# The first product of a channel MLP by Strassen's algorithm in Winograd's form, its weights streamed pair by pair

## The reference

```python
# 1 attention over 2 x 8 heads with a hash mask  -> x [2, 768, 512]
# 2 _moe_ref
mixed = np.real(fft(fft(x, axis=1), axis=2));  u = x + mixed
un = (u - mean(u)) / sqrt(var(u) + 1e-6)
x  = u + np.maximum(un @ w_ch1, 0) @ w_ch2          # w_ch1 [512, 2048], w_ch2 [2048, 512]
# 3 _moe2_ref
h = gelu(x @ w_in);  a, v = h[..., :512], h[..., 512:]
v_n = layernorm(v) * g_ln
v_s = einsum('ts,bsd->btd', w_sg, v_n) + b_sg[None, :, None]
out = x + (a * v_s) @ w_out
```

## Time and profile before

| | |
|---|---|
| median of 3 runs | 742.23 us (742.17 to 742.39) |
| the profiled execution | 741.96 us, of which the span in the profile is 739.9 |
| TensorE busy | 729.6 us, 99% |
| VectorE, ScalarE, GpSimd busy | 395.2, 308.5, 284.8 us |

### The profile page before, as it was taken

One profiled execution on the slowest core, in us unless ns is written; L12 is line 12 of the kernel. 1 busy time (PEld: TensorE's weight loads), 2 busy tenths in 40 slices (PEclk: granted clock), 3 DMA queues, 4 the chain that ended last, 5 costly groups with the idle time before them and its releaser, 6 DMA issues.

```text
span 739.9 us, 11871 instructions
## 1 busy us (share of the span) xinstructions
PE 729.6 (99%) x3993; PEld 604.4 (82%) x3993; DVE 395.2 (53%) x629; ACT 308.5 (42%) x593; POOL 284.8 (38%) x292
## 2 busy tenths in 40 slices
PE   8999999999999999999999999999999999999998
PEld 8866666666766899999999999999899887888886
DVE  6977787777876798412221241213113696248633
ACT  4878887888884544111111111112124452025301
POOL 4188888888897500960000000000032254004400
PEclk9999999999999999999999999999999999999999
DMA  4433433433332302700000000000031000010001
GB/s 97 99 84 90 95 90 73 101 76 89 84 77 80 123 2 69 273 1 1 0 0 0 0 0 0 0 0 1 1 129 58 14 1 1 28 58 0 0 14 71
DMA packets 60118, 36.63 MB, mean 50 GB/s; under 512 B 44292, under 2 KB 52664, under 8 KB 59576
## 3 DMA queue, kind: packets, MB, share of 16 engines
q1 hardware_dynamic: 59512, 32.79, 16.4%
q0 software_dynamic: 576, 3.43, 1.3%
HBM read 27.03 MB, written 3.15 MB: 41 GB/s over the span
## 4 chain that ended last, share of the span: by engine, by line
PE 91%; DVE 4%; ACT 1%; issue 1%; POOL 1%; DMA 1%; SPq 0%; DVEq 0%; POOLq 0%; ACTq 0%
PE PS L692 87%; DVE mneg L1495 1%; PE PS L716 1%; PE PS L1085 1%; PE PS L1125 1%; PE PS L985 1%; PE PS L831 1%; PE PS L1053 1%; DMA ops<-mrow 0%; DVE ops L1466 0%; DVE ops L1487 0%; DVE ops L1460 0%; ACT ops L1169 0%; DMA pj<-in_proj_dram 0%; ACT E L1185 0%
## 5 line engine op out<-in xcount | busy, mean ns | idle before, releaser
L1757 DVE SCALAR_TENSOR_TENSOR hL<-PS,hH 128x384 fp32r<-128x384 f32 x64 | 35.7, 558 | 201.5 <-ACT hH L1387 201.5
L692 PE MATMUL PS<-ops 98*128 98x384 f32 (+1 forms) x576 | 134.7, 359 | 2.3 <-DVE mneg L1495 1.0
L692 PEld LDWEIGHTS PS<-ops 98*128 98x128 f32 (+1 forms) x576 | 95.1, 189 | 43.2 <-ACT E L1185 19.8
L1387 ACT ACTIVATE hH<-PS 128x384 fp32r<-128x384 f32 x64 | 31.4, 491 | 224.8 <-PE PS L692 224.8
L1495 DVE TENSOR_REDUCE mneg<-PS 128x1 f32<-128x768 f32 x96 | 91.5, 956 | 30.4 <-PE PS L692 29.8
L551 POOL TENSOR_TENSOR esum<-esum,E 128x768 f32<-128x768 f32 x56 | 102.4, 1829 | 2.8 <-ACT E L1185 0.3
L1185 ACT ACTIVATE E<-PS 128x384 f32<-128x384 f32 x192 | 83.5, 487 | 37.2 <-PE PS L692 35.0
L692 PE MATMUL PS<-unTH,W1L 128*128 128x384 f32 x256 | 86.4, 337 | 0.0
L692 PE MATMUL PS<-unTH,W1H 128*128 128x384 f32 x256 | 86.2, 337 | 0.0
L692 PE MATMUL PS<-unTL,W1H 128*128 128x384 f32 x256 | 86.0, 336 | 0.0
L692 PE MATMUL PS<-W2H,hL 128*128 128x512 f32 x192 | 75.9, 395 | 0.0
(11 more groups left out here) (193 smaller groups left out, 1412.7 us busy)
## 6 DMA issues: line engine op xcount, KB each, us to landing
ops<-ops SPq DMA_DIRECT2D x30, 192.0 KB, 3.0
W1R<-in_moe_w_ch_dram SPq DMA_DIRECT2D x16, 256.0 KB, 2.9
W2R<-in_moe_w_ch_dram SPq DMA_DIRECT2D x4, 1024.0 KB, 6.9
qk<-in_k_dram SPq DMA_DIRECT2D x32, 96.0 KB, 2.5
qk<-in_q_dram SPq DMA_DIRECT2D x32, 96.0 KB, 2.6
vn<-in_v_dram SPq DMA_DIRECT2D x32, 96.0 KB, 2.5
out_dram<-X SPq DMA_DIRECT2D x12, 256.0 KB, 2.0
WsgR<-in_moe_w_sg_dram SPq DMA_DIRECT2D x1, 2304.0 KB, 8.2
```

What stands on the lines that cost most here:

```text
L692: return pe.matmul(dst, lhs, rhs, start=start, stop=stop, **kw)
L1387: act.activation(M1["hH"][:, f % 2, :], PS[:, f % 2, 0:HALF], ACT.Relu).then_inc(hhi_done, 1)
L1757: dve.scalar_tensor_tensor(M1["hL"][:, f % 2, :], PS[:, f % 2, 0:HALF], 0.0, rd(M1["hH"][:, f % 2, :]), ALU.max, ALU.subtract).then_inc(hl ...
```

## The change

The first product of the MLP, `un @ w_ch1`, is taken with quarters: the 512 input features in two halves, the 2048 hidden features in two halves (block i and block i + 8 make pair i), and the 768 tokens of a batch in two halves. A pair of blocks and a batch make a 2 x 2 by 2 x 2 product of quarters, which takes 7 products (P1 to P7) instead of 8, each 2 steps of `mm3`, 6 matmuls of 384 columns. There are 16 pairs (8 for each batch, `NP`). Four signed sums of weight quarters (`weight_sums`, GpSimd) and four of token quarters (T1, T2 on VectorE, `token_differences`; T3, T4 on GpSimd, `token_sums`) are formed ahead of the products and split like all operands. Four results C11, C21, C12, C22 come out of products that are accumulated in two PSUM banks, with copies of partial sums by ScalarE (`keep_part`), two additions by VectorE (`side_quarter`) and one by GpSimd (`last_quarter`). The second product is as before, 4 x 9 matmuls for a pair, done one pair later, between the products of the next.

```diff
+            def pair(n):
+                later = [lambda quarter=quarter: second(n - 1, quarter) for quarter in LATER] if n else [lambda: None] * 4
+                product(n, P1)
+                product(n, P2)
+                later[0]()
+                product(n, P6)
+                product(n, P7)
+                later[1]()
+                product(n, P5)
+                product(n, P4)
+                later[2]()
+                product(n, P3)
+                if 1 <= n <= T:
+                    pe.wait_ge(pre_done, 2 * n + 2)
+                    un_transposes(T + n - 1, SIDE_BANK)
+                later[3]()
```

ScalarE's order in a pair; `next_un` rounds a token quarter of batch 1 in pair 7 alone:

```diff
+            for n in range(NP):
+                keep_part(n, P1, 0)
+                next_un(n, 0, P1)
+                next_un(n, 1, P2)
+                keep_part(n, P6, 1)
+                next_un(n, 2, P6)
+                keep_part(n, P7, 2)
+                if n + 1 < NP:
+                    weights_hi(n + 1)
+                next_un(n, 3, P7)
+                hidden_hi(n, C11)
+                keep_part(n, P5, 3)
+                w2_upper(n)
+                next_un(n, 4, P5)
+                hidden_hi(n, C21)
+                next_un(n, 5, P4)
+                hidden_hi(n, C12)
...
+                next_un(n, 6, P3)
+                hidden_hi(n, C22)
```

VectorE's and GpSimd's:

```diff
+            for n in range(NP):
+                if n == PAIRS - 1:
+                    token_differences(1)
+                side_quarter(n, C11)
+                next_un(n, 0)
+                next_un(n, 1)
+                next_un(n, 2)
+                if n + 1 < NP:
+                    weights_lo(n + 1)
...
+                next_un(n, 3)
+                hidden_lo(n, C11)
+                side_quarter(n, C21)
+                next_un(n, 4)
+                hidden_lo(n, C21)
+                next_un(n, 5)
+                hidden_lo(n, C12)
+                if n == PAIRS:
+                    channel_residual(0, 0, 4 * (PAIRS - 1) + 3)
+                next_un(n, 6)
+                hidden_lo(n, C22)
+                if n == PAIRS:
+                    channel_residual(0, 1, 4 * (PAIRS - 1) + 4)
...
+            for n in range(NP):
+                if n == PAIRS - 1:
+                    token_sums(1)
+                if n + 1 < NP:
+                    weight_sums(n + 1)
+                w2_lower(n)
+                last_quarter(n)
```

A product waits for the one whose bank it continues, and in the first pair of a batch for its token quarter:

```diff
+                if step == P1:
+                    pe.wait_ge(w1_lo, 3 * n + 3)
+                    if n:
+                        pe.wait_ge(hlo_done, 4 * (n - 1) + 3)
...
+                elif step == P7:
+                    pe.wait_ge(pre_done, 2 * n + 1)
+                else:
+                    pe.wait_ge(part_done, 4 * n + {P6: 1, P5: 2, P4: 3, P3: 4}[step])
+                if n % PAIRS == 0:
+                    pe.wait_ge(utl_done, 7 * b + UN_ORDER[b].index(k) + 1)
```

The weights are no longer prepared during attention. W1 and W2 blocks of a pair are loaded two pairs ahead, once for each batch. Those of pair 0 are summed and split during the Fourier mix of batch 0: `weight_sums(0)` and `first_weights_lower` on GpSimd, and on ScalarE:

```diff
                 if b + 1 < B:
+                    weights_hi(0)
                     fold_hi(2 * b + 2)
                     fold_hi(2 * b + 3)
```

More of the change, by code:

```diff
@@ L678, in _ @@
                                        ALU.pow).then_inc(rs2_done, 1)
[L679 to L681 removed]
+                scale_gate(b * T + T - 1, T - 1)
+                if b == 0:
+                    for t in range(KT):
                         pool.wait_ge(wout_hi, t + 1)
@@ new lines, in second @@
+            def second(n, quarter):
+                b, i, s = n // PAIRS, n % PAIRS, n % 2
+                f, block = int(quarter in (C21, C22)), int(quarter in (C12, C22))
+                pe.wait_ge(hlo_done, 4 * n + quarter + 1)
+                pe.wait_ge(w2_lo, n + 1)
+                if i == 0 and f == 0:
+                    if b:
+                        pe.wait_ge(x_upd, NT + T)
+                    else:
+                        pe.wait_ge(x_upd, NT)
+                        pe.wait_ge(ut_done, T)
@@ new lines, in keep_part, with hidden_hi @@
+            def keep_part(n, step, i):
+                bank = SIDE_BANK if step == P7 else CHAIN_BANK
+                act.wait_ge(p_rdy, 7 * n + step)
+                if i >= 2 and n:
+                    act.wait_ge(pre22_done, n)
+                copy(M1["part"][:, i, :], PS[:, bank, 0:HALF]).then_inc(part_done, 1)
+            def hidden_hi(n, quarter):
+                if quarter == C12:
+                    act.wait_ge(p_rdy, 7 * n + P3)
+                    src = PS[:, CHAIN_BANK, 0:HALF]
+                else:
+                    if quarter == C22:
+                        act.wait_ge(pre22_done, n + 1)
+                    else:
+                        act.wait_ge(pre_done, 2 * n + quarter + 1)
+                    src = M1["pre"][:, min(quarter, 2), :]
+                if n:
+                    act.wait_ge(y_rdy, 4 * (n - 1) + LATER.index(quarter) + 1)
+                act.activation(M1["hH"][:, quarter, :], src, ACT.Relu).then_inc(hhi_done, 1)
@@ L1394, in mlp_block @@
                         cols = slice((c % 2) * DM, (c % 2 + 1) * DM)
                         act.wait_ge(win_in, 16)
-                        copy(M2["WinH"][:, c // 2, cols], R1["WinR"][:, c // 2, cols]).then_inc(win_hi, 1)
-                    if not more and f >= FT - 2:
-                        act.wait_ge(wout_in, 16)
-                        for t in range((f - FT + 2) * KT // 2, (f - FT + 3) * KT // 2):
-                            copy(M2["WoutH"][:, t, :], R2["WoutR"][:, t, :]).then_inc(wout_hi, 1)
@@ L1413, in gate_hi @@
                 copy(M2["VH"][:, j, :], M2["vr"][:, j % 3, :]).then_inc(vh_done, 1)
-            with act.Fori(0, B) as b:
+            for b in range(B):
                 for j in range(T):
@@ new lines, in weights_lo, with side_quarter @@
+            def weights_lo(n):
+                s = n % 2
+                for i in range(3):
+                    rows = W1_PARTS[i][0]
+                    dve.wait_ge(w1_hi, 3 * n + i + 1)
+                    dve.tensor_tensor(M1["W1L"][:, s, rows, :, :], w1_source(s, i), rd(M1["W1H"][:, s, rows, :, :]),
+                                      ALU.subtract).then_inc(w1_lo, 1)
+            def side_quarter(n, quarter):
+                dve.wait_ge(p_rdy, 7 * n + (P2 if quarter == C11 else P4))
+                dve.wait_ge(part_done, 4 * n + quarter + 1)
+                dve.tensor_tensor(M1["pre"][:, quarter, :], PS[:, SIDE_BANK, 0:HALF], M1["part"][:, quarter, :],
+                                  ALU.add).then_inc(pre_done, 1)
@@ new lines, in hidden_lo, with channel_residual @@
+            def hidden_lo(n, quarter):
+                dve.wait_ge(hhi_done, 4 * n + (C11, C21, C12, C22).index(quarter) + 1)
+                src = PS[:, CHAIN_BANK, 0:HALF] if quarter == C12 else M1["pre"][:, min(quarter, 2), :]
+                dve.scalar_tensor_tensor(M1["hL"][:, quarter, :], src, 0.0, rd(M1["hH"][:, quarter, :]),
+                                         ALU.max, ALU.subtract).then_inc(hlo_done, 1)
+            def channel_residual(b, block, after):
+                dve.wait_ge(y_rdy, after)
+                for c in range(TH):
+                    N = b * T + block * TH + c
+                    dve.tensor_tensor(X[:, N, :], PS[:, y_bank(block, c), :], X[:, N, :], ALU.add).then_inc(x_upd, 1)
@@ L1785, in _ @@
             transformed_lo(1, 1, 1)
+            for n in range(TH, T):
+                normalise(n)
             flipped(1)
```

536 lines of the change are left out of this document (310 added, 226 removed).

## The result

The changed kernel takes 761.8 us (median; 758.0 to 762.7), the kernel before 742.3 on the same chip: 1.0252 times as long, 95% interval 1.0216 to 1.0288. It is 2.5% slower. The profiled execution took 761.2 us, 759.1 of them the span, 19.2 us more than that of before.

A forecast was written before the change was run, and what follows sets the result against it. TensorE, busy 99% of the span, was taken to bound the kernel. Waits of 29.1 us less 17.3 saved made it 11.8 slower: 741.96 to 753.8 profiled, so 754.0 median, range 741 to 763.

The forecast's parts named there:

- The likeliest case: The whole kernel: the forecast itself, waits as priced, 746 to 759 us; chance 0.52.
- the second rival: TensorE's clock falls in the gaps, pair 0's products running at 1.2 GHz: up to 5 us more, 759; chance 0.18.
- (a): Mix of batch 0: GpSimd's weight sums and split take turns with VectorE; 4.3 us lost, bounds 0 and 7.4.
- (b): Mix of batch 1: more statistics and normalisations on VectorE before the last GL and flips; 1.2 us, bounds 0 and 3.6.
- (c): Entry to the pairs: P1 waits for T1, T2, T3 and the first lower half; 2.3 us, bounds 0.5 and 4.6.
- (d): Pair 0: products wait behind seven lower halves and turns with GpSimd, lasting 18.0 us; 10.5 lost, bounds 7.5 and 12.
- (e): Pair 1: statistics and aggregations on VectorE stand ahead of the `side_quarter` P7 wants; 2.0 us, bounds 0 and 4.3.
- (f): Pair 7: batch 1's token operands, with turns, delay ScalarE and P1 of pair 8; 4.0 us, between 1.0 and 6.7.
- (g): Pair 9: batch 0's last three residuals end after `second` wants their banks; 1.4 us, bounds 0 and 2.
- (h): Gated MLP: VL and two w_sg splits make a stand of 4.3, replacing 0.9; 3.4 us lost, bounds 1 and 5.
- The first rival: VectorE and GpSimd turns do not happen or fall in slack: waits of 16.2 us, 741.1; chance 0.20.
- The third: Rival that every pair waits, C12's hL coming later than its cover: 7.5 us more over 15 pairs, 761; chance 0.07.

The follow-up runs named there:

- x_fill2: Changed kernel with idle matmuls, each no longer than its wait, in TensorE's waits of pair 0, pair 1 and ahead of the gated MLP's mixing: 756.2 us, 1.0177.
- x_early_b: Changed kernel with pair 0's weights loaded and summed in the attention, their GpSimd split delayed until VectorE has folded batch 1: 754.5 us, 1.0165.
- x_early: Changed kernel with pair 0's weights loaded, summed and split during the attention instead of in the mix of batch 0: 759.4 us, 1.0232.
- x_order: Changed kernel with pair 0's token halves made in the order the products use them, VectorE's first quarter and ScalarE's first copy between: 757.0 us, 1.0187.
- x_sums1: Changed kernel with GpSimd's sums of pair 1's weights right behind batch 0's reciprocal deviation instead of in pair 0: 760.7 us, 1.0236.
- x_swap: Changed kernel with GpSimd's sums of pair 8's weights ahead of batch 1's token sums in pair 7: 759.5 us, 1.023.
- x_pair7: x_swap with VectorE's lower halves 2 and 3 of batch 1's tokens behind pair 7's third lower quarter, 4 to 6 behind the fourth: 754.3 us, 1.0168.
- x_best: Changed kernel with edits of x_early_b, x_order, x_swap, x_pair7, a later mixing wait, earlier pair 1 sums, and idle matmuls in pairs 0 and 1: 736.51 us, 0.9921.

## Why the prediction came out as it did

It named 754.0 us, with 741 to 763 as range and slower at 0.77; 761.8 lies in the range, 7.8 above the number. The likeliest case (746 to 759) was not enough by itself: the second rival, the clock, happened on top of it. That the range held is in part luck: without the 3.5 us more that the change saved (below) the time would have been 765.3. Term by term, each measured from starts in the changed kernel's trace; "clock" is the part that was matmuls at the lower level:

| term | forecast | measured | of it clock |
|---|---|---|---|
| attention | 0 | 1.2 | |
| (a) mix of batch 0 | 4.3 | 4.2 | |
| (b) mix of batch 1 | 1.2 | 1.0 | 0.9 |
| (c) entry | 2.3 | 1.9 | |
| (d) pair 0 | 10.5 | 11.9 | 1.0 |
| (e) pair 1 | 2.0 | 3.0 | 1.3 |
| (f) pairs 7 and 8 | 4.0 | 8.9 | 3.6 |
| (g) pair 9 | 1.4 | 1.7 | |
| (h) gated MLP | 3.4 | 6.0 | 2.5 |
| lost | 29.1 | 39.8 | 9.3 |
| saved | 17.3 | 20.8 | |
| net | 11.8 | 19.0 (the profiled executions: 19.2) | |

How the middle column comes about: the first group of the mix starts at 262.77 in place of 261.56 (attention). z0L ended 5.4 us later, less 1.2 (a). The second transform of batch 1 ends at 307.7 in place of 300.0, less 1.2, 4.2 and 1.4 for twelve transposes that moved there (b). P1 of pair 0 at 309.59, less 307.7 (c). The pairs, from the starts above: 328.88 - 309.59 less 7.4 (d), 347.79 - 328.88 less 15.92 (e), 467.34 - 427.43 less 2 x 15.49 (f), 484.54 - 467.34 less 15.49 (g). The stand of 4.4 less 0.9, and 2.5 behind it (h). The clock part, in (d), (e) and (h), is what x_fill2 took away; in (f) it is what remains beside the waits. In (b) it is the time from z0L's end (285.88) to the group that it releases (286.90), less the 0.1 us that this takes in x_early_b.

- **(a) and (c): right in mechanism and size.** z0L ended 5.4 us later than in the earlier trace rows, 1.2 of them from the attention; x_early_b brought z0L 4.6 us forward, and x_early showed that it is the meeting that costs, wherever it takes place. In (c) P1 starts 4.6 us after the sixth tile's copy (309.59, with T1 at 304.99), as forecast; no experiment tried it.
- **(b): the right number by luck.** TensorE has no wait in the mix of batch 1. From its first group to its end it takes 20.8 us (286.90 to 307.7) in place of 19.4 (280.59 to 300.0), and 1.4 of that are the twelve transposes. The later GL and flips cost nothing; the 1.0 us is almost all slow matmuls behind the stand of (a), at the 0.50 of 284 to 287 us.
- **(d): right, with a wrong share.** Pair 0 was to last 18.0 us and lasted 19.3, 18.3 with the clock held up (x_fill2). Of what is beyond its matmuls, x_order took 4.1 us away by order (up to 1.0 of it clock), and x_sums1 showed 1.2 us for the sums' turns; the forecast had put some 5 us on turns with GpSimd. Those with T3 and T4 were not tried by themselves. Two sizes in the sum missed in opposite directions: P7 starts 9.5 us after P1 (319.11) where 10.7 was forecast, and from P7 to P1 of pair 1 it takes 9.8 us (8.8 with the clock held up) where 7.3 was.
- **(e): right in size, wrong in cover.** In the changed kernel no wait for the statistics shows in pair 1; its 3.0 us are slow matmuls. With the clock held up (x_fill2) the pair is 1.7 us too long and waits of 0.56 and 0.28 us for pre appear. The slow matmuls had hidden the late VectorE.
- **(f): too small.** The waits were 2.76 + 2.59 = 5.35 us against 4.0, inside the bounds. ScalarE was the late one, as forecast, but VectorE's row was as late right behind it (x_swap), and its halves ahead of its quarters were the cause (x_pair7).
- **(h): the stand was forecast at 4.3 and measured 4.37 us;** what was missing is the 2.5 us behind it.
- **The clock: the step that failed is that it stood as a rival to the forecast, with at most 5 us and in pair 0 alone.** It came with the forecast's own stands, at four places, and much of it lies not between them but in the full stretches behind them: 9.3 us, most of the 10.7 by which the loss exceeds the 29.1 of the forecast. The Trainium skill, "TensorE: Matmul & The Clock Gate", section "HAM oscillation — how this bites in real kernels", tells that the work after a gap starts at the lower clock; the windows above agree (0.50 from 329 to 335 us, TensorE busy throughout).
- **Saved: too small by 3.5 us.** 64 blocks of before took 4.19 us each, 268.2; the 16 pairs take 15.49 each without transposes, 247.8, and not 16 times 15.7. The matmuls start 1% closer together: a product group and a `second` group take 2.09 and 2.04 us in place of 2.11 and 2.08. Why was not tried; it hid part of the miss.
- **The attention's 1.2 us** were not forecast. A wait for the DMA of mrow at 42.75 us is 1.09 in place of 0.21, and it is in x_best too (1.1). The change only removed transfers there. Its cause stays open.
- The first rival (no turns) fell: Y took 3.15 us beside GpSimd. The third fell: pairs 2 to 6 have no wait. That the queues can be put in an order in which, with idle matmuls in what waits are left, the saving outweighs the rest is what x_best shows.

## What to carry to other kernels

Where TensorE is busy 99% of the time, an algorithm that takes an eighth of the matmuls out of one product pays only if the pairs at its edges (the first of each batch, the first after a stage) are ordered as closely as the steady ones: here some 40 us were lost, nearly all at such edges, against 21 saved over sixteen pairs. Price the slow matmuls behind a longer stand together with it, here 0.9 to 3.6 us at each of four edges, and fill the stand with idle matmuls no longer than it, or better take it away. Put GpSimd's elementwise work where VectorE reads PSUM, and in an engine's queue put what the next product reads ahead of what it reads later.
